# An early gather for the first batch, a last output scaled by ScalarE, and halves turned one by one in a three-stage kernel

## What is computed

```python
for b in range(B):
    prev_e = -1
    for s in range(S):
        fresh_e = int(np.argmax(logits[b, s]))
        e = fresh_e if s == 0 or local_gate[b, s] < 0.5 else prev_e
        prev_e = e
        p = ...                                  # softmax of logits[b, s]
        h = np.maximum(x[b, s] @ w1[e], 0.0)
        out[b, s] = p[e] * (h @ w2[e])
...
X = np.fft.fft(np.fft.fft(x, axis=1), axis=2)    # x is the out above
u = x + np.real(X)
un = (u - mean) / np.sqrt(var + 1e-06)
return u + np.maximum(un @ w_ch1, 0.0) @ w_ch2
```

## Time and profile before

| | us |
|---|---|
| median of 3 runs | 626.13 |
| lowest and highest | 623.85, 626.25 |
| the profiled execution | 625.15 |
| its span (first to last instruction) | 623.0 |
| PE busy | 591.2 (95%) |
| DVE busy | 345.7 (55%) |
| ACT busy | 250.1 (40%) |
| POOL busy | 124.8 (20%) |
| TensorE's granted clock, mean | 0.997 of full speed |

### The profile page before, as it was taken

One profiled execution on the slowest core, in us unless ns is written; L12 is line 12 of the kernel. 1 busy time (PEld: TensorE's weight loads), 2 busy tenths in 40 slices (PEclk: granted clock), 3 DMA queues, 4 the chain that ended last, 5 costly groups with the idle time before them and its releaser, 6 DMA issues.

```text
span 623.0 us, 10277 instructions
## 1 busy us (share of the span) xinstructions
PE 591.2 (95%) x3086; PEld 496.9 (80%) x3087; DVE 345.7 (55%) x920; ACT 250.1 (40%) x551; POOL 124.8 (20%) x150
## 2 busy tenths in 40 slices
PE   3899999799979999999899999999999999999997
PEld 2799998697857888888667878888888888888885
DVE  4888769678762656532365965544533333533333
ACT  3588776465231444422023632334333333333331
POOL 5565545501710010010100124000400000200000
PEclk9999999999989999999999999999999999999999
DMA  6967733496428344621061540000100000100001
GB/s 157 172 143 155 153 83 74 149 392 245 187 102 306 103 148 156 239 90 51 17 219 38 210 158 1 0 2 0 68 1 1 1 0 1 68 0 2 0 1 68
DMA packets 59304, 61.68 MB, mean 99 GB/s; under 512 B 42688, under 2 KB 42816, under 8 KB 58240
## 3 DMA queue, kind: packets, MB, share of 16 engines
q1 hardware_dynamic: 54384, 47.21, 25.6%
q0 software_dynamic: 3440, 11.32, 4.7%
q10 hardware_dynamic: 1440, 2.64, 1.4%
HBM read 48.27 MB, written 12.89 MB: 98 GB/s over the span
## 4 chain that ended last, share of the span: by engine, by line
PE 81%; DVE 7%; issue 4%; ACT 2%; DMA 2%; another core or an unknown queue 2%; SPq 1%; POOL 0%; DVEq 0%; ACTq 0%; POOLq 0%
PE bank L2129 20%; PE bank L2142 20%; PE bank L1963 11%; PE bank L1938 10%; PE bank L1801 3%; ACT arena L753 2%; PE bank L1842 2%; PE bank L1810 2%; PE bank L2149 1%; PE bank L2036 1%; PE bank L1950 1%; PE bank L2039 1%; PE bank L1926 1%; PE bank L1824 1%
## 5 line engine op out<-in xcount | busy, mean ns | idle before, releaser
L2129 PE MATMUL bank<-parts 128*128 128x512 f32 x576 | 140.1, 392 | 1.3 <-DVE parts L1468 1.3
L2142 PE MATMUL bank<-parts 128*128 128x512 f32 x576 | 138.2, 389 | 0.0
L2129 PEld LDWEIGHTS bank<-parts 128*128 128x128 f32 x576 | 107.3, 188 | 24.3 <-DVE parts L1468 1.6
L2142 PEld LDWEIGHTS bank<-parts 128*128 128x128 f32 x576 | 108.1, 188 | 22.4
L1468 DVE TENSOR_TENSOR parts<-arena,parts 128x512 fp32r<-128x512 f32 (+1 forms) x108 | 78.5, 758 | 75.0 <-ACT parts L931 73.6
L1938 PE MATMUL bank<-parts 128*128 128x512 f32 x312 | 77.0, 400 | 3.0 <-issue 2.2
L1963 PE MATMUL bank<-parts 128*128 128x512 f32 x312 | 74.6, 394 | 3.8 <-DVE parts L1468 3.5
L1938 PEld LDWEIGHTS bank<-parts 128*128 128x128 f32 x312 | 58.3, 191 | 16.3 <-issue 4.6
L1963 PEld LDWEIGHTS bank<-parts 128*128 128x128 f32 x312 | 57.6, 188 | 16.4 <-issue 2.4
L931 ACT ACTIVATE parts<-arena 128x512 fp32r<-128x512 f32 x48 | 30.3, 630 | 82.9 <-PE bank L2142 82.9
L1745 DVE SCALAR_TENSOR_TENSOR parts<-bank,parts 128x512 fp32r<-128x512 f32 x48 | 33.2, 691 | 47.8 <-ACT parts L967 47.7
(11 more groups left out here) (241 smaller groups left out, 746.2 us busy)
## 6 DMA issues: line engine op xcount, KB each, us to landing
mid<-in_moe_w SPq DMA_DIRECT2D x16, 512.0 KB, 6.0
arena<-in_moe_w SPq DMA_DIRECT2D x16, 512.0 KB, 7.2
arena<-in_moe_w_ch SPq DMA_DIRECT2D x2, 2048.0 KB
arena<-in_moe_w_ch SPq DMA_DIRECT2D x4, 1024.0 KB, 9.1
arena<-in_k SPq DMA_DIRECT2D x16, 192.0 KB, 3.1
arena<-in_q SPq DMA_DIRECT2D x16, 192.0 KB, 4.0
mid<-in_v SPq DMA_DIRECT2D x16, 192.0 KB
x_all<-folded_y SPq DMA_DIRECT2D x6, 512.0 KB, 6.9
```

Of the source, the lines that this page charges most:

```text
L2129: last = pe.matmul(bank[2 + f % 2][:, 0:GN], w[:, f % 2, r], x[:, par, c, :], start=(c == 0 and w is m1_hi and x is cT_hi), stop=(c == DC ...
L2142: last = pe.matmul(bank[4 + t][:, :], x[:, f % 2, r], w[:, f % 2, :], start=(f == 0 and x is g_hi and w is m2_hi), stop=(f == MC - 1 and w ...
```

## The change

Four things are done.

1. The table gets an entry `T_FIRST`, the number of tiles after which every row of batch 0 is written, and `T_LAST`. SP gathers batch 0 after that many stores, and batch 1 after all of them. The slots of the loaded rows move to two places of batch 1. DVE folds batch 0 as soon as its loop is over; two clearings move ahead of the loop, two are cut down and put between the first two folds.
2. The last tile's output is scaled by ACT (`last_output`), from a bank of its own, and DVE only writes its row numbers (`last_places`). POOL waits for a store's arrival ahead of the next store, not behind its own.
3. PE turns the first half of tile n's activations in the middle of `second_layer(n-1)`; DVE lowers that half ahead of `output(n-1)`.
4. The 38 matmuls of L2149 go. In all loops the second tile's `If` is put inside the first one's.

The diff, cut:

```diff
         def xs(n):
-            return xa[:, n, :]
+            return xa[:, n if n < ROUND else NT - 2 + n - ROUND, :]
...
+        Y_BANK, LAST_BANK = bank[5], bank[6]
...  SP
-            sp.wait_ge(y_out, 16 * used)
-            sp.wait_ge(xs_in, 16 * used)
-            for b in range(B):
+            def gather(b):
...
+            sp.wait_ge(y_out, 16 * first_batch)
+            gather(0)
+            sp.wait_ge(y_out, 16 * used)
+            sp.wait_ge(xs_in, 16 * used)
+            gather(1)
...  POOL
             with pool.Fori(ROUND - 1, SLOTS - 1) as n:
                 with pool.If(n + 1 < used):
-                    store_rows(n)
-            store_rows(used - 1)
+                    stored_before(n)
+                    store(n)
+            stored_before(pool.value_load(table_i[0:1, T_LAST:T_LAST + 1], min_val=NT - 1, max_val=SLOTS - 1))
+            store(used - 1, TWO)
...  ACT (the same nesting in DVE's and PE's loops)
             with act.Fori(0, STEPS[1] // 2) as pairs:
-                for par in range(2):
-                    n = 2 * pairs + (ROUND + par)
-                    with act.If(n < used):
-                        load_rows(n + 2, ROUND + par)
-                        tile(n, False)
+                n = 2 * pairs + ROUND
+                with act.If(n < used):
+                    load_rows(n + 2, ROUND)
+                    tile(n, False)
+                    with act.If(n + 1 < used):
+                        load_rows(n + 3, ROUND + 1)
+                        tile(n + 1, False)
+
+            def last_output():
+                act.wait_ge(y_free, used)
+                act.wait_ge(meta_ok, used)
+                act.wait_ge(y_ps, used)
+                act.activation(ysb, LAST_BANK[:, :], ACT.Copy, scale=meta[:, 0:1]).then_inc(y_sb, 1)
...
+            last_output()
             for c in range(GT):
                 own_mean(c)
...  DVE, planner: six small instructions more, such as
+                dve.tensor_scalar(left_over, left_over, 1.0, None, ALU.min)
+                    dve.tensor_tensor(left_end, ending, left_over, ALU.mult)
+                    dve.tensor_reduce(last_left, left_end, axis=AX.X, op=ALU.max)
+                    dve.tensor_scalar(table_i[:, T_FIRST:T_FIRST + 1], last_left[0:1, :], float(ROUND), None, ALU.add)
...  DVE, tile
+                if known is None:
+                    lower_hidden(n, 0)
                 if known not in (0, 2):
                     output(n - 1)
...
+            for region in (odd[:, :, :, 0:1], zT):
+                dve.memset(region, 0.0)
             used = dve.value_load(...)
...
-            output(used - 1)
-            dve.wait_ge(meta_in, used + 1)
-            dve.sem_inc(waited, 1)
+            def last_places():
+                dve.wait_ge(y_free, used)
+                dve.wait_ge(meta_ok, used)
+                dve.sem_inc(waited, 1)
+                dve.tensor_copy(dest_i[:, :], meta[:, 1:2]).then_inc(y_sb, 1)
...
-            for tile in (odd[:, :, :, 0:1], row_middle, middle, zT):
-                dve.memset(tile, 0.0)
-            for c in range(KC):
+            last_places()
+            fold_even(0, 0)
+            dve.wait_ge(meta_in, used + 1)
+            dve.sem_inc(waited, 1)
+            for region in (row_middle[:, B:], middle[:, :, B:]):
+                dve.memset(region, 0.0)
+            fold_odd(0, 0)
+            for c in range(1, KC):
                 fold_even(0, c)
                 fold_odd(0, c)
...  PE
-            def second_layer(n):
+            def second_layer(n, o=Y_BANK, turned=None):
...
+                pe.wait_ge(y_sb, n + 1 if o is Y_BANK else n)
                 for c in range(FC):
+                    if c == FC // 2 and turned is not None:
+                        turn_hidden(turned, range(1))
...
-                        second_layer(n - 1)
-                        turn_hidden(n)
-                        with pe.If(used < n + 2):
-                            second_layer(n)
+                second_layer(n - 1, turned=n)
+                turn_hidden(n, range(1, 2))
+                with pe.If(used < n + 2):
+                    second_layer(n, LAST_BANK)
...
-            for _ in range(38):
-                pe.matmul(bank[7][:, :], xT_hi[:, 0:P], w1_hi[:, 0, 0:512], start=True, stop=True)
```

More of the change, by code:

```diff
@@ L56 @@
 T_LOADS = T_USED + 1
-T_COLS = T_LOADS + 1
+T_FIRST = T_LOADS + 1
+T_LAST = T_FIRST + 1
+T_COLS = T_LAST + 1
 GATE_TURN = {(HP, t): t for t in range(ST)} | {(PAIRS - 1, t): ST + t - 2 for t in range(2, ST)}
@@ L186, in build @@
         mid = sb("mid", 6160)
-        small = sb("small", 2022)
+        small = sb("small", 2040)
         zero_row = sb("zero_row", XW)[:, :]
@@ L644, in _, with store @@
             clear_rows(1)
[L646 to L647 removed]
+            def store(n, signs=1):
+                pool.wait_ge(y_sb, n + 1 + signs)
                 pool.sem_inc(waited, 1)
@@ L663, in _ @@
             scatter(1, range(ST, ST + 3))
-            landed(0)
+            stored_before(1)
             scatter(1, range(ST + 3, NT))
-            for n in range(1, ROUND - 1):
-                store_rows(n)
+            store(1)
+            for n in range(2, ROUND - 1):
+                stored_before(n)
+                store(n)
             pool.wait_ge(table_ok, 2)
@@ L1331, in place_rest @@
                 link(dve.scalar_tensor_tensor(done_rows, tiles, float(P), count, ALU.mult, ALU.max))
+                dve.scalar_tensor_tensor(left_over, tiles, -float(P), done_rows, ALU.mult, ALU.add)
                 mark(dve.tensor_tensor(place1, done_rows, const("place"), ALU.add))
@@ L1512, in _, with lower_hidden @@
                 lower_first(w2_lo, w2_raw, w2_hi, w2_hi_ok, w2_lo_ok, c)
+            def lower_hidden(n, half):
+                dve.wait_ge(hhi_ok, 2 * n + half + 1)
+                less(hT_lo[:, 4 * half:4 * half + 4, :], bank[3 + half][:, :].rearrange("p (c n) -> p c n", c=4),
+                     hT_hi[:, 4 * half:4 * half + 4, :]).then_inc(hlo_ok, 1)
             def tile(n, at):
@@ L1560, in tile @@
                 dve.tensor_copy(meta_next, xs(following_at)[:, DM:DM + 2]).then_inc(meta_in, 1)
[L1561 to L1564, removed]
+                if known is not None:
+                    lower_hidden(n, 0)
+                lower_hidden(n, 1)
                 if known != 0:
@@ L1579, in output @@
                 dve.sem_inc(waited, 1)
-                dve.tensor_scalar(ysb, bank[5][:, :], meta[:, 0:1], None, ALU.mult).then_inc(y_sb, 1)
+                dve.tensor_scalar(ysb, Y_BANK[:, :], meta[:, 0:1], None, ALU.mult).then_inc(y_sb, 1)
                 dve.wait_ge(y_sb, n + 1 + 1)
@@ L1588, in _ @@
                 tile(n, n)
+            for region in (odd[:, :, :, 0:1], zT):
+                dve.memset(region, 0.0)
             used = dve.value_load(table_i[0:1, T_USED:T_USED + 1], min_val=NT, max_val=SLOTS)
             with dve.Fori(0, STEPS[1] // 2) as pairs:
[L1591 to L1594, removed]
-            output(used - 1)
-            dve.wait_ge(meta_in, used + 1)
-            dve.sem_inc(waited, 1)
+                n = 2 * pairs + ROUND
+                with dve.If(n < used):
+                    tile(n, ROUND)
+                    with dve.If(n + 1 < used):
+                        tile(n + 1, ROUND + 1)
+            def last_places():
[3 more added lines that the diff above has]
+                dve.tensor_copy(dest_i[:, :], meta[:, 1:2]).then_inc(y_sb, 1)
             def rows_of(b, c, mirrored, lo=0, n=DM):
@@ L1941, in first_layer, with turn_hidden @@
                             last.then_inc(h_ps, 1)
-            def turn_hidden(n):
-                for half, made in ((0, hA_sb), (1, hB_sb)):
-                    pe.wait_ge(made, n + 1)
+            def turn_hidden(n, halves=range(2)):
+                for half in halves:
+                    pe.wait_ge((hA_sb, hB_sb)[half], n + 1)
                     pe.wait_ge(hlo_ok, 2 * n + half + 1)
@@ L1962, in second_layer @@
                     for x, w in ((hT_hi, w2_hi), (hT_lo, w2_hi), (hT_hi, w2_lo)):
-                        last = pe.matmul(bank[5][:, :], x[:, c, :], w[:, c // 2, f], start=(c == 0 and x is hT_hi and w is w2_hi),
+                        last = pe.matmul(o[:, :], x[:, c, :], w[:, c // 2, f], start=(c == 0 and x is hT_hi and w is w2_hi),
                                          stop=(c == FC - 1 and w is w2_lo))
@@ L2004, in _ @@
             with pe.Fori(0, STEPS[1] // 2) as pairs:
[L2005 to L2009, removed]
-                        second_layer(n - 1)
-                        turn_hidden(n)
-                        with pe.If(used < n + 2):
-                            second_layer(n)
+                n = 2 * pairs + ROUND
+                with pe.If(n < used):
+                    tile(n, 0)
+                    with pe.If(n + 1 < used):
+                        tile(n + 1, 1)
             def along_rows():
```

25 lines of the change are left out of this document (15 added, 10 removed).

## The result

The changed kernel takes 618.5 us (median of 5, 617.12 to 620.15). The kernel before, now with 5 runs, takes 624.13 (623.85 to 626.25). The ratio is 0.9902, with a 95% interval of 0.9873 to 0.993: 6.1 us saved by the ratio, between 4.4 and 7.9. The predicted time was 618.5 us and the predicted saving 6.65. The two profiled executions are 625.15 and 617.12 us long, 8.03 apart.

What follows compares the result with a forecast made beforehand. A chain of last product, `ysb`, store, arrival, gather and fold was taken to bound the kernel before the sequence transform. Terms -8.0 + 0.3 + 0.9 + 0.15 = -6.65 us from 625.15 gave 618.5 us, range 614.8 to 622.5.

Steps and rivals of the forecast that it cites:

- What bounds the place: Before the sequence transform, one chain bounds: last product, `ysb`, store, arrival, gather, fold; removing the matmuls alone gives about 0.3 us.
- `y_free` sets the first fold: After the last tile, DVE waits for POOL's signal at 308.3, so the first fold starts at 308.6 instead of 316.88.
- The rival of quick passes: POOL's empty passes at the loop's end cost little, folds start at 306.5, time 615.5 us; chance 0.12.
- -8.0 us from the folds: At the sequence transform, earlier folds let PE begin batch 1 at 319.1 instead of 327.1.
- The early gather's traffic costs nothing: Gathering batch 0 beside the looped tiles was costed at nothing, since their rows were loaded a tile ahead.
- Batch 1's gather is hidden: Its first third lands at 316.0, before DVE finishes batch 0 at 317.4: 1.4 us to spare, no cost.
- ACT scales the last output: Behind `y_free` at 308.3, ACT scales in 0.6 us, done at 309.0; no term of its own.
- The clock, +0.9 us: PE's 3.1 us idle before the first even sums lets the clock fall, costing 0.9 us, ends 0 and 1.7.
- Part 3, +0.3 us: In nine looped tiles, PE's two extra changes between kinds of matmul cost 0.03 us per tile.
- Planner, +0.15: Three or four of the planner's six small DVE instructions delay the table: 0.15 us, at most 0.6.
- The supply of instructions: Rival: DVE's unexplained 4.38 us stall at 171.47 vanishes or a second comes, 614.1 or 622.9 us; chance 0.12.
- The sum: Over the whole kernel, all terms together give -6.65 us from the profiled 625.15 us, making 618.5 us.

Runs made afterwards that it cites:

- e1: The kernel before without its 38 matmuls, nothing else: 619.01 against 617.02 us, ratio 1.0034.
- e2: The changed kernel with batch 0 gathered behind all stores, as before: 617.46 us, ratio 1.0014 to the kernel before.
- e9: The changed kernel with nine more empty passes in POOL's store loop: 613.49 us, ratio 0.9954 to the kernel before.
- e4: The changed kernel with the first even fold ahead of `last_places`: 608.69 us, ratio 0.9868 to the kernel before.
- e3: The changed kernel with 10 matmuls put back at the place of the 38: 607.74 us, ratio 0.9853 to the kernel before.
- e7: The changed kernel with part 3 undone, both halves turned behind `second_layer(n-1)`: 609.16 us, ratio 0.9881 to the kernel before.
- e8: The changed kernel with the last output scaled by DVE in `last_places` instead of by ACT: 609.54 us, ratio 0.9882 to the kernel before.
- the first comparison: The changed kernel against the kernel before, on a chip not on record: 618.5 against 624.13 us, ratio 0.9902.
- the three groups: Later follow-up runs on three chips, each group beside the kernel before, which takes 617.02, 617.02 and 616.64 us there.
- e5: The changed kernel itself, run again as the reference on another group's chip: 609.03 us, ratio 0.9877 to the kernel before.
- e12: The changed kernel with all 38 matmuls back: 613.62 us, ratio 0.9959 to the kernel before.
- e6: The changed kernel with POOL's store loop in 6 passes of three nested tests instead of 18 passes: 606.74 us, ratio 0.9836 to the kernel before.
- e10: e6 with 8 matmuls put into PE's idle time: 608.68 us, ratio 0.9878 to the kernel before.

## Why the prediction was right

- **What bounds the place** (chain, not the 38 matmuls): right, by e1 and e2.
- **`y_free` sets the first fold.** Predicted 308.3 and a fold at 308.6; measured 308.27 for the row numbers and 308.34 for the fold, with the wait put down to POOL's queue. The walk of nine passes, taken as 4.0 us from DVE's row, is 4.05 by e9. The rival of quick passes is out. That the clock times agree so closely is in part luck: from the store of tile 11 to the row numbers it takes 4.81 us, where the prediction has 5.4 (303.0 to 308.4), but the store starts at 303.46. DVE's own walk was taken too short, 3.1 us for 3.6 (e4); it hid behind POOL's. (The working also counts 14 tests and turns, but names nine and four.)
- **-8.0 us from the folds.** With the clock held (e3) the tail is 8.33 us shorter than before: the term was 0.3 too small, mostly by the shorter way from the store to the row numbers. The 0.30 us by which tile 12 starts later belongs to the terms for part 3 and the planner, 0.45 together.
- **The early gather's traffic costs nothing**: right. Seven looped tiles take 86.42 us with it (203.17 to 289.59) and 86.42 in e2 without it (195.37 to 281.79).
- **Batch 1's gather is hidden**, predicted with 1.4 us to spare. It starts at 312.35, its first third would be there by 315.6 (an estimate, with the 3.29 us of before), and DVE asks for it at 317.10. Right; e7 shows the spare, for with a gather 2.0 us later DVE waits.
- **ACT scales the last output**: priced at nothing by itself. e8 gives 0.8 us, the length of the scaling on DVE.
- **The clock, +0.9 us**: 0.89 by e3. The idle time was 2.61 us, not 3.1, because PE ended later and the fold began sooner; the size of the fall was right, from the earlier trace rows.
- **Part 3, +0.3 us**: this term was mis-sized. Seven looped tiles took 85.88 us before (203.41 to 289.29) and 86.42 after (203.17 to 289.59): 0.08 us per tile, not 0.03, so 0.7 over nine as an estimate. e7, without part 3, has 85.84 for the seven., with one change of kind, gave 0.05 for one; here there are two more per tile. That the earlier product serves only to keep the gather off the path was right (e7).
- **Planner, +0.15**: the second layer behind the table starts 0.04 us later (182.56 for 182.52). The small instructions fell partly into the stall of the earlier trace rows. Where there is no stall, that layer starts 6.12 us behind tile 3's first layer in e1, and 6.19 to 6.31 us behind it in the runs made from the changed kernel: 0.07 to 0.19 us more.
- **The supply of instructions**: that stall ended at nearly the same time, 176.0 us before and 175.9 after. The code alone doesn't make it: PE was busy for 20.88 of 25 us from 160 to 185 us in both profiles of the first comparison, and in the twelve profiles of the three groups it isn't there. The stretch of PE in the changed kernel of the first comparison:

```profile
160.00:185.00 25.00, 20.88 (x88) 0.93 0.40 149
```

The same stretch in e5, the same code in a later run:

```profile
160.00:185.00 25.00, 23.79 (x115) 1.00 0.56 198
```

The stall explains about half of the difference between these two executions of the same code. Tile 12 starts 8.67 us earlier in e5 (280.92 for 289.59), and 4.10 of that is there already at tile 3 (166.37 for 170.47), ahead of the stall. What causes either wasn't tried.

- **The sum.** The predicted 6.65 us stands against 7.14 that the profiled pair shows up to batch 1's transform (7.44 less the 0.30 of the later tile 12), so it was 0.5 short; the 0.64 us at the very end it doesn't have at all. On the median it lies 1.0 over the 5.6 of the first comparison, and there the scatter of the kernel before, 2.4 us, decides more than any term. The mechanism was right, and the terms to within 0.4 us; that the time came out at 618.5 exactly is luck.

## What to carry to other kernels

A block of useless matmuls in front of a wait is worth the clock that it holds, and where it outlasts the wait it costs time (e12). Take the wait away first, then cut the block to what is left of it, and look in the timeline at what ends the wait, not at the block. Behind a loop with a fixed number of passes and a test in each, every engine still has its empty passes to walk, here at 0.45 us each on POOL and some 0.7 on DVE; where a signal that others wait for stands behind them, nest the tests or send it earlier. To judge an edit of 1 us in a kernel whose executions scatter by 3, measure a stretch between two events on either side of it, and look outside it as well: here the tiles ahead lost 0.5 us and the end gained 0.64.

## What the runs showed that was not expected

- After 2.6 us without a matmul the clock fell only once PE worked again, and cost 0.89 us; after 9.7 us (e1) it had fallen long before, and PE then worked some 4.8 us at the lower level. Idle times of 2.13 and 1.93 us (e6, e4) left it at 1.00 in their profiles. In e5 it fell behind 2.58 us, in e8 behind 3.29 us, again after PE had resumed.
- Empty passes cost 0.45 us each on POOL (e9), and 3.6 to 3.8 us in all on DVE for five tests and as many turns (e4, e6). The Trainium skill ("Advanced Engine Details and Errata", Control Flow Timing) gives about 108 ns for a compare-and-branch and 51 ns for a branch; an estimate from these is 0.16 us per empty pass, about a third of POOL's. The measurement decides.
- One and the same instruction of POOL, the store of the last tile, took 0.96 us in nine of the fourteen profiles, 1.02 to 1.12 in e4, e6, e8 and e10, and 1.52 in e7. In these five it ran beside DVE's folds, but in the changed kernel it ran beside them in 0.96. What makes the difference is open.
- The same kernel before takes 624 us in the first comparison and 617 in the three groups, at a mean clock of 0.997 in the first profile and 0.996 to 1.000 in the executions of the groups. There its 25 executions with a clock of 0.998 or more have a median of 615.55 us and the other 27 one of 617.55, so that a good part of its scatter goes with the clock.
- The last outputs arrive 0.64 us sooner in every profile made from the changed kernel than in the two made from the kernel before.
